# A triangular solve regrouped: four diagonal blocks of 8 rows and two levels of merging in place of two blocks of 16

## The chip, the cores and the metric

The kernel runs on one core of a Trainium2 chip. The metric is the device time of one launch in microseconds. The kernel before took 894.9 us, the median of three runs (891.95 to 898.2).

## What is computed

Three stages one after another: a delta-rule attention over 4 batches, 8 heads and 768 tokens of width 48, then a gated MLP without a nonlinearity, then a second MLP with SoLU and a layer norm.

```python
# attention, for each batch and head
k_n = k / (norm(k) + 1e-06)
for t in range(S):
    kt, vt, bt = k_n[t], v[t], beta[t]
    y[t] = q[t] @ state
    v_old = state.T @ kt
    state = state + bt * outer(kt, vt - v_old)
# first MLP:  x = ((x @ w1) * (x @ w2)) @ w3 @ w_out
# second MLP: h = x @ w_in; solu = h * softmax(h); layer norm * g; @ w_out
```

The loop over tokens is computed in chunks of 64 tokens. Inside a chunk the corrections of all tokens hang on one another through a lower triangular matrix, so each chunk needs the inverse of a unit lower triangular system. That inverse, made in halves of 32 rows, is what the change touches.

## The kernel before

**Tiles and groups.** The sequence is cut into six groups (NG = 6) of two chunks of 64 tokens. One group holds 32 systems (8 heads, 2 batch pairs, 2 chunks), and the two batches of a pair and the two 32-row halves of a chunk lie on the four quarters of the partitions. So one operation on a tile of 128 partitions by 32 x 32 elements works on the inverses of the whole group. Group 0 stands before the hardware loop, groups 1 to 4 are its two iterations of two groups, and group 5 stands behind it. In this attention stage the first MLP's products are already computed from the chunk before (`up` on TensorE, `keep_a` on ScalarE, `multiply` on VectorE), so they fill the engine between the steps of the recurrence.

**Two halves of a group.** Each group has two halves, one for each chunk (tt = 0 and tt = 1). On TensorE (`group`, L868) a half is: `k_state` (L767) for both pairs, `up` 0, `apply_inverse` of the first 32 rows, `up` 1, `cross_half`, `up` 2, `apply_inverse` of the second 32 rows, `up` 3, `outputs`, `up` 4, `add_state`, `up` 5, `outputs`, `up` 6, `add_state`, two `transpose_y`, `up` 7. In the first half the four `grams` of the next group stand between these. `k_state` waits at L772 for the semaphore `x_low` (written by `low_x`, L466, on VectorE), because it writes the PSUM banks from which `low_x` reads. `up` f waits at L847 for the `product` of `multiply` f-2. `apply_inverse` of the first half waits once a group for `inverse`.

**VectorE's queue.** It is written out by hand in `group` (L486): an engine works strictly in this order. In the first half it multiplies f = 0 to 3 and keeps the masked scores (`keep_pt`); behind the fourth `keep_pt` stand `coefficients` and `system_rows` of the next group's solve, and then the solve itself, cut into pieces between which the multiplications stand. In the first half these are rows 1 to 3, multiply 4, rows 4 to 6, multiply 5, rows 7 and 8, multiply 6, rows 9 and 10, both `low_x`, multiply 7; in the second half `right_hand`, rows 11 and 12, multiply 0, rows 13 to 15, multiply 1, `right_hand2`, and then the four pieces of merging and `stationary`, with multiplications 2 to 6 between, then both `low_x` and multiply 7. The solve of group 0 stands in one run before the groups (L573 to L579), and group 0 has no multiplications in its first half.

**The solve.** `system_rows` (L385) transposes the 32 x 32 Gram blocks (`amat`) and scales the rows with the coefficients `ci` and -1 (L390, 1024 elements). `substitute` (L394) solves two diagonal blocks of 16 rows at once: row i takes one product over 2 x i x i elements (L402) and one sum over them (L404), each waiting for the one before. `below_first` (L411) and `below_second` (L423) fill the lower left 16 x 16 block as -X22 A21 X11, in two parts each, of 1024 and 2048 products (L417, L429) with a sum behind each (L421, L433). In L429 the innermost index runs down a column of `xt`, in steps of 32 elements. `stationary` (L435) multiplies by `ci` (L439, 1024 elements) and transposes into `ti`, which `apply_inverse` reads.

Of the kernel before, what the change touches and what calls it, by code (L numbers as in the profile page):

```python
# [8 lines left out]
ALU = mybir.AluOpType  # L9
ACT = mybir.ActivationFunctionType  # L10
AX_X = mybir.AxisListType.X
# [5 lines left out]
P = 128  # L17
# [3 lines left out]
QB = HB // 2  # L21
NP = B // 2
# [72 lines left out]
def attention(nc, sb, sem, ps, m_dram, w34_dram, kq, ktok, vtok, beta, w1, w2, w3t, wo1,  # L95
# [11 lines left out]
    with ExitStack() as mem:  # L107
# [32 lines left out]

        zt = gd[:, 0:QB * QB // HB, :].rearrange("p s (a j) -> p (s a) j", j=QB)
        ksq = tmp[:, 0:SYS * D].rearrange("p (s d) -> p s d", d=D)
# [77 lines left out]

        GCOEF, GSOLVE = 4, 2 * (QB - 1) + 8 + 4

# [76 lines left out]
        def _(pool):  # L299
# [17 lines left out]
            const(pool.memset(xt[:, :, :].rearrange("p k j -> p (k j)")[:, 0:HB * HB:HB + 1], 1.0))  # L317
# [38 lines left out]
        def _(dve):  # L356
            def blocks(mat, first, *dims):

                a = mat[:, :, :]
                return bass.AP(a.tensor, a.offset + first, [list(a.ap[0]), [QB * HB + QB, 2], *dims])  # L360
# [48 lines left out]
            E8 = QB // 2  # L409

            def below_first(n, k0, j0, part):  # L411

                nj = QB - j0
                t = tmp[:, 0:QB * E8 * nj].rearrange("p (k i j) -> p k i j", k=E8, j=nj)
                step = GSOLVE * n + 3 + 2 * (QB - 1) + 2 * part
                dve.wait_ge(solve, step)
                dve.tensor_tensor(t, amat[:, QB:HB, j0:QB].unsqueeze(1).to_broadcast([P, E8, QB, nj]),  # L417
                                  xt[:, k0:k0 + E8, j0:QB].unsqueeze(2).to_broadcast([P, E8, QB, nj]),
                                  ALU.mult).then_inc(solve, 1)
                dve.wait_ge(solve, step + 1)  # L420
                dve.tensor_reduce(zt[:, k0:k0 + E8, :], t, AX_X, ALU.add).then_inc(solve, 1)  # L421

            def below_second(n, i0, nj, part):  # L423

                t = tmp[:, 0:QB * E8 * nj].rearrange("p (k i j) -> p k i j", k=QB, j=nj)
                x22 = xt[:, QB:QB + nj, QB + i0:QB + i0 + E8].rearrange("p j i -> p i j")
                step = GSOLVE * n + 3 + 2 * (QB - 1) + 2 * part
# [1006 lines left out]
```

## Time and profile before

| | us |
|---|---|
| median of three runs (lowest, highest) | 894.9 (891.95, 898.2) |
| span of the profiled execution | 894.6 |
| PE (TensorE matmul) busy | 819.3 |
| DVE (VectorE) busy | 524.4 |
| ACT (ScalarE) busy | 363.4 |
| POOL (GpSimd) busy | 62.9 |

Spans and starts are microseconds from the first instruction of the profiled execution. L402 is line 402 of the kernel. An idle time stands with the instruction that ends it, and with the one that released it. The attention stage reaches to about 540 us; groups 1 to 4 lie between 150 and 462 us.

### The profile page before, as it was taken

To read this page: it belongs to the slowest core of one execution; us is meant where nothing else is said; L and a number is where in the kernel's file an instruction comes from. 1 tells how busy PE (TensorE), PEld (TensorE's weight loads), DVE (VectorE), ACT (ScalarE), POOL (GpSimd) and SP (SyncE) were. 2 spreads that over 40 slices of the span, in tenths; PEclk is the share of its full clock that TensorE was granted. 3 is DMA by queue.
4 is the path that set the end of the run, shared out by engine and by line. 5 is a ranking of instruction groups with operands and counts; after the bars stand their busy time and mean duration, and the time that the engine had idled before them with its cause. 6 is when DMAs were issued, how large, how long until landed. Compare 5 with 4: busy or idle time off the path is not lost. (4 is left out here: it accounts for less than half of the span.)

```text
span 894.6 us, 22766 instructions
## 1 busy us (share of the span) xinstructions
PE 819.3 (92%) x9324; PEld 735.9 (82%) x9324; DVE 524.4 (59%) x859; ACT 363.4 (41%) x753; POOL 62.9 (7%) x102
## 2 busy tenths in 40 slices
PE   3869699999999899999999997999979999999995
PEld 2537588989889798988989996778869999999995
DVE  4794677379378837957872213444335566565663
ACT  2704522723453262354333323253334444444442
POOL 3410100010010001001000000000000000000000
PEclk9979888999899899999999999999999999999999
DMA  8772302220402221140011133756000000000000
GB/s 207 242 190 75 81 14 75 95 58 29 143 14 73 72 97 41 48 143 26 27 37 38 37 113 116 236 172 208 5 1 18 20 25 18 23 21 20 25 18 27
DMA packets 41226, 65.39 MB, mean 73 GB/s; under 512 B 3248, under 2 KB 31024, under 8 KB 39984
## 3 DMA queue, kind: packets, MB, share of 16 engines
q1 hardware_dynamic: 39120, 59.36, 22.6%
q10 hardware_dynamic: 2016, 4.72, 1.7%
q8 instruction: 70, 1.15, 0.5%
q14 instruction: 20, 0.16, 0.1%
HBM read 45.19 MB, written 18.87 MB: 72 GB/s over the span
## 5 line engine op out<-in xcount | busy, mean ns | idle before, releaser
L672 ACT COPY asb<-ps 128x256 f32<-128x256 f32 x96 | 35.7, 372 | 203.4 <-PE ps L852 203.1
L483 DVE TENSOR_TENSOR msb<-asb,ps 128x256 f32<-128x256 f32 x96 | 40.2, 419 | 91.0 <-ACT asb L672 90.6
L1361 PE MATMUL ps<-woh,uth 128*128 128x384 f32 x192 | 65.9, 343 | 2.6 <-DVE utl L1254 2.6
L852 PE MATMUL ps<-xh,w1h 128*128 128x256 f32 x288 | 61.4, 324 | 7.4 <-DVE msb L483 7.4
L1361 PE MATMUL ps<-woh,utl 128*128 128x384 f32 x192 | 65.8, 343 | 0.0
L1361 PE MATMUL ps<-wol,uth 128*128 128x384 f32 x192 | 65.6, 341 | 0.0
L1107 PE MATMUL ps<-mh,w34h 128*128 128x512 f32 x144 | 58.1, 403 | 7.0 <-DVE ml L1076 7.0
L763 PE MATMUL ps<-kqs,kbd 112*128 112x128 f32 x384 | 50.0, 287 | 12.3 <-ACT kbd L609 12.3
L763 PEld LDWEIGHTS ps<-kqs,kbd 112*128 112x128 f32 x384 | 48.4, 203 | 14.9 <-ACT kbd L609 13.8
L382 DVE TENSOR_TENSOR pt<-ps,mask 128x512 f32<-128x512 f32 x24 | 16.6, 690 | 71.9 <-ACT a L623 71.9
L1254 DVE TENSOR_TENSOR utl<-ps,uth 128x512 fp32r<-128x512 f32 x48 | 30.9, 686 | 45.2 <-ACT uth L1300 45.2
L1107 PE MATMUL ps<-ml,w34h 128*128 128x512 f32 x144 | 57.4, 399 | 0.0
L1107 PE MATMUL ps<-mh,w34l 128*128 128x512 f32 x144 | 57.3, 398 | 0.0
L1286 ACT ACTIVATE e<-ps,nmax 128x1024 f32<-128x1024 f32 x24 | 26.8, 1116 | 67.3 <-DVE nmax L1221 67.3
L852 PE MATMUL ps<-xh,w2h 128*128 128x256 f32 x288 | 52.6, 294 | 0.0
L852 PEld LDWEIGHTS ps<-xh,w1h 128*128 128x128 f32 x288 | 41.9, 196 | 12.5 <-DVE msb L483 7.9
L852 PE MATMUL ps<-xl,w2h 128*128 128x256 f32 x288 | 52.2, 292 | 0.0
L852 PE MATMUL ps<-xh,w1l 128*128 128x256 f32 x288 | 52.0, 291 | 0.0
L852 PE MATMUL ps<-xl,w1h 128*128 128x256 f32 x288 | 51.7, 290 | 0.0
L852 PE MATMUL ps<-xh,w2l 128*128 128x256 f32 x288 | 51.2, 288 | 0.0
L630 ACT COPY uu<-ps 32x384 f32<-32x384 f32 x96 | 45.1, 470 | 7.2 <-PE ps L789 5.8
L1227 DVE SCALAR_TENSOR_TENSOR u<-ps,e 128x1024 f32<-128x1024 f32 x24 | 29.4, 1224 | 31.8 <-ACT e L1286 31.8
(134 smaller groups left out, 1904.3 us busy)
## 6 DMA issues: line engine op xcount, KB each, us to landing
m_dram<-msb SPq DMA_DIRECT2D x48, 256.0 KB, 2.1
kqs<-in_kq SPq DMA_DIRECT2D x24, 384.0 KB, 6.2
mrest<-m_dram SPq DMA_DIRECT2D x36, 256.0 KB, 5.4
ks<-in_ktok SPq DMA_DIRECT2D x6, 768.0 KB, 7.7
vs<-in_vtok SPq DMA_DIRECT2D x6, 768.0 KB, 9.0
out<-osb SPq DMA_DIRECT2D x24, 192.0 KB
mfirst<-m_dram SPq DMA_DIRECT2D x12, 256.0 KB, 5.0
rr<-in_w SPq DMA_DIRECT2D x8, 192.0 KB, 4.4
```

Source lines behind the costliest of these rows:

```text
L382: dve.tensor_tensor(pt[:, par, tile, :, :], gbank[:, :, C:P], mask[:, :].unsqueeze(1).to_broadcast([P, H, C]), ALU.mult).then_inc(pt_made, 1)
L483: dve.tensor_tensor(msb[:, f // 2 % 2, f % 2, :], asb[:, f % 2, :], bbank[f % 2], ALU.mult).then_inc(product, 1)
L630: ins = act.copy(uu[rows, g, :], chain[g][rows, :])
L672: act.copy(asb[:, f % 2, :], abank[f % 2]).then_inc(a_kept, 1)
L763: ins = pe.matmul(gbank[:, h, :], kbd[:, tile % 2, h, :], kqs[:, par, tile, h, :], start=True, stop=True)
L852: ins = pe.matmul(bank, w[:, k, cols], xx[:, par, k, :], start=(j == 0 and k == 0), stop=(j == 2 and k == KD - 1))
L1107: ins = pe.matmul(hbank[par][k], w[:, f, k * P:(k + 1) * P], mm[:, u, f % UF, :, :].rearrange("p t c -> p (t c)"), start=(f == 0 and j == ...
L1227: dve.scalar_tensor_tensor(out=u[:, s, :], in0=hb[s], scalar=1.0, in1=e[:, :], op0=ALU.mult, op1=ALU.mult, accum_out=us[:, s:s + 1]).then_ ...
L1254: dve.tensor_tensor(utl[:, j, :, :], tb[j].rearrange("p (k c) -> p k c", c=P), uth[:, j, :, :].bitcast(F32), ALU.subtract).then_inc(ut_low, 1)
L1286: act.activation(e[:, :], hb[s], ACT.Exp, bias=nmax[:, s:s + 1], accum_out=es[:, s:s + 1]).then_inc(expd, 1)
L1361: ins = pe.matmul(ob, xx[:, j, k, :], w[:, 4 * j + k, :], start=(j == 0 and k == 0 and p == 0), stop=(j == 1 and k == 3 and p == 2))
```

## The change

The diagonal is solved in four blocks of 8 rows at once (`substitute` for rows 1 to 7, 4 x i x i elements each). Two new pieces, `eights_first` and `eights_second`, merge pairs of them to 16 rows; the merging to 32 rows stays. The sign moves into the sums (`negate=True`). The scaling by `ci` at the end (L439) is gone: `ci` is copied onto the diagonal of `xt` instead (32 elements), and the scaling at the start covers the diagonal 8 x 8 blocks only (256 elements). In `below_second` the products are laid out with the former inner index outside, so that the product reads in unit steps and the sum behind it reads in steps of 8 elements (32 bytes). GpSimd no longer writes ones onto the diagonal of `xt`. In VectorE's queue the pieces of the solve stand in other places: all seven rows, `eights_first` and `eights_second` now stand in the first half, ahead of both `low_x`, and rows 11 to 15 are gone from the second half.

```diff
 QB = HB // 2
+EB = QB // 2
...
         zt = gd[:, 0:QB * QB // HB, :].rearrange("p s (a j) -> p (s a) j", j=QB)
+        z8 = gd[:, 0:QB * QB // HB, :].rearrange("p s j -> p (s j)")[:, 0:QB * EB].rearrange(
+            "p (b k i) -> p b k i", b=2, k=EB)
...
-        GCOEF, GSOLVE = 4, 2 * (QB - 1) + 8 + 4
+        DIAG8, DIAG16 = EB * HB + EB, QB * HB + QB
+        MERGED8 = 4 + 2 * (EB - 1) + 7
+        GCOEF, GSOLVE = 4, MERGED8 + 8
...
             const(pool.memset(xt[:, :, :], 0.0))
-            const(pool.memset(xt[:, :, :].rearrange("p k j -> p (k j)")[:, 0:HB * HB:HB + 1], 1.0))
             const(pool.memset(st[:, :, :], 0.0))
...
             def system_rows(n):
+
                 dve.wait_ge(gram_kept, TPG * (n + 1))
                 dve.transpose(amat[:, :, :], gd[:, :, :].rearrange("p s i -> p i s")).then_inc(solve, 1)
+                if not static_below(n, 1):
+                    dve.wait_ge(inverse, n)
+                dve.wait_ge(solve, GSOLVE * n + 1)
+                dve.tensor_copy(steps_of(xt, 0, [HB + 1, HB]), ci[:, :]).then_inc(solve, 1)
                 dve.wait_ge(solve, GSOLVE * n + 2)
-
-                dve.scalar_tensor_tensor(out=amat[:, :, :], in0=amat[:, :, :], scalar=-1.0,
-                                         in1=ci[:, :].unsqueeze(2).to_broadcast([P, HB, HB]),
-                                         op0=ALU.mult, op1=ALU.mult).then_inc(solve, 1)
+                rows = steps_of(amat, 0, [DIAG8, HB // EB], [HB, EB], [1, EB])
+                dve.tensor_tensor(rows, rows, steps_of(ci, 0, [EB, HB // EB], [1, EB], [0, EB]),
+                                  ALU.mult).then_inc(solve, 1)
 
             def substitute(n, rows):
 
-
                 for i in rows:
-                    xs = blocks(xt, 0, [HB, i], [1, i])
-                    t = tmp[:, 0:2 * i * i].rearrange("p (b k j) -> p b k j", b=2, j=i)
-                    arow = blocks(amat, i * HB, [0, i], [1, i])
-                    dve.wait_ge(solve, GSOLVE * n + 3 + 2 * (i - 1))
+                    t = tmp[:, 0:4 * i * i].rearrange("p (b k j) -> p b k j", b=HB // EB, j=i)
+                    xs = steps_of(xt, 0, [DIAG8, HB // EB], [HB, i], [1, i])
+                    arow = steps_of(amat, i * HB, [DIAG8, HB // EB], [0, i], [1, i])
+                    dve.wait_ge(solve, GSOLVE * n + 4 + 2 * (i - 1))
                     dve.tensor_tensor(t, xs, arow, ALU.mult).then_inc(solve, 1)
-                    dve.wait_ge(solve, GSOLVE * n + 4 + 2 * (i - 1))
-                    dve.tensor_reduce(blocks(xt, i, [HB, i]), t, AX_X, ALU.add).then_inc(solve, 1)
-
...
+                    dve.wait_ge(solve, GSOLVE * n + 5 + 2 * (i - 1))
+                    dve.tensor_reduce(steps_of(xt, i, [DIAG8, HB // EB], [HB, i]), t, AX_X,
+                                      ALU.add, negate=True).then_inc(solve, 1)
+
+            def eights_first(n):
+
+                step = GSOLVE * n + 4 + 2 * (EB - 1)
+                t = tmp[:, 0:2 * EB * EB * EB].rearrange("p (b k i j) -> p b k i j", b=2, k=EB, j=EB)
+                dve.wait_ge(solve, step)
+                for b in range(2):
+                    at = b * DIAG16
+                    dve.tensor_tensor(t[:, b], steps_of(amat, at + EB * HB, [0, EB], [HB, EB], [1, EB]),
+                                      steps_of(xt, at, [HB, EB], [0, EB], [1, EB]), ALU.mult).then_inc(solve, 1)
+                dve.wait_ge(solve, step + 2)
+                dve.tensor_reduce(z8[:, :, :, :], t, AX_X, ALU.add).then_inc(solve, 1)
+
+            def eights_second(n):
+
+                step = GSOLVE * n + 4 + 2 * (EB - 1) + 3
+                t = tmp[:, 0:2 * EB * EB * EB].rearrange("p (b k j i) -> p b k j i", b=2, k=EB, j=EB)
+                dve.wait_ge(solve, step)
+                for b in range(2):
+                    x22 = steps_of(xt, b * DIAG16 + EB * HB + EB, [0, EB], [HB, EB], [1, EB])
+                    dve.tensor_tensor(t[:, b], x22, z8[:, b].unsqueeze(3).to_broadcast([P, EB, EB, EB]),
+                                      ALU.mult).then_inc(solve, 1)
+                dve.wait_ge(solve, step + 2)
+                for b in range(2):
+                    dve.tensor_reduce(steps_of(xt, b * DIAG16 + EB, [HB, EB], [1, EB]),
+                                      t[:, b].rearrange("p k j i -> p k i j"), AX_X, ALU.add,
+                                      negate=True).then_inc(solve, 1)
...
             def below_second(n, i0, nj, part):
 
-                t = tmp[:, 0:QB * E8 * nj].rearrange("p (k i j) -> p k i j", k=QB, j=nj)
-                x22 = xt[:, QB:QB + nj, QB + i0:QB + i0 + E8].rearrange("p j i -> p i j")
-                step = GSOLVE * n + 3 + 2 * (QB - 1) + 2 * part
+                t = tmp[:, 0:QB * EB * nj].rearrange("p (k j i) -> p k j i", k=QB, i=EB)
+                x22 = xt[:, QB:QB + nj, QB + i0:QB + i0 + EB]
+                step = GSOLVE * n + MERGED8 + 2 * part
                 dve.wait_ge(solve, step)
-                dve.tensor_tensor(t, x22.unsqueeze(1).to_broadcast([P, QB, E8, nj]),
-                                  zt[:, :, 0:nj].unsqueeze(2).to_broadcast([P, QB, E8, nj]),
+                dve.tensor_tensor(t, x22.unsqueeze(1).to_broadcast([P, QB, nj, EB]),
+                                  zt[:, :, 0:nj].unsqueeze(3).to_broadcast([P, QB, nj, EB]),
                                   ALU.mult).then_inc(solve, 1)
                 dve.wait_ge(solve, step + 1)
-                dve.tensor_reduce(xt[:, 0:QB, QB + i0:QB + i0 + E8], t, AX_X, ALU.add).then_inc(solve, 1)
+                dve.tensor_reduce(xt[:, 0:QB, QB + i0:QB + i0 + EB], t.rearrange("p k j i -> p k i j"), AX_X,
+                                  ALU.add, negate=True).then_inc(solve, 1)
 
             def stationary(n, par):
 
-                t = tmp[:, 0:HB * HB].rearrange("p (j i) -> p j i", i=HB)
-                dve.wait_ge(solve, GSOLVE * (n + 1) - 1)
-                dve.tensor_tensor(t, xt[:, :, :], ci[:, :].unsqueeze(2).to_broadcast([P, HB, HB]),
-                                  ALU.mult).then_inc(solve, 1)
                 dve.wait_ge(solve, GSOLVE * (n + 1))
                 dve.transpose(ti[:, par, :, :].rearrange("p s i -> p i s"),
-                              t.rearrange("p j i -> p i j")).then_inc(inverse, 1)
+                              xt[:, :, :].rearrange("p j i -> p i j")).then_inc(inverse, 1)
...
@@ -510,19 +537,18 @@
                     keep_pt(n + 1, nxt, 3)
                     coefficients(n + 1, nxt)
                     system_rows(n + 1)
-                    substitute(n + 1, range(1, 4))
                 if up0:
                     multiply(half, 4)
                 if ahead:
-                    substitute(n + 1, range(4, 7))
+                    substitute(n + 1, range(1, EB))
                 if up0:
                     multiply(half, 5)
                 if ahead:
-                    substitute(n + 1, range(7, 9))
+                    eights_first(n + 1)
                 if up0:
                     multiply(half, 6)
                 if ahead:
-                    substitute(n + 1, range(9, 11))
+                    eights_second(n + 1)
                 low_x(n, 0, 0)
...
                 right_hand(n, par, 1, 0)
                 right_hand(n, par, 1, 1)
-                if ahead:
-                    substitute(n + 1, range(11, 13))
                 multiply(half, 0)
-                if ahead:
-                    substitute(n + 1, range(13, QB))
                 multiply(half, 1)
                 right_hand2(n, 1, 0)
                 right_hand2(n, 1, 1)
                 if ahead:
-                    below_first(n + 1, E8, E8, 0)
+                    below_first(n + 1, EB, EB, 0)
                 multiply(half, 2)
                 if ahead:
                     below_first(n + 1, 0, 0, 1)
                 multiply(half, 3)
                 if ahead:
-                    below_second(n + 1, 0, E8, 2)
+                    below_second(n + 1, 0, EB, 2)
                 multiply(half, 4)
                 if ahead:
-                    below_second(n + 1, E8, QB, 3)
+                    below_second(n + 1, EB, QB, 3)
                 multiply(half, 5)
                 if ahead:
                     stationary(n + 1, nxt)
...
             system_rows(0)
-            substitute(0, range(1, QB))
-            below_first(0, E8, E8, 0)
+            substitute(0, range(1, EB))
+            eights_first(0)
+            eights_second(0)
+            below_first(0, EB, EB, 0)
             below_first(0, 0, 0, 1)
-            below_second(0, 0, E8, 2)
-            below_second(0, E8, QB, 3)
+            below_second(0, 0, EB, 2)
+            below_second(0, EB, QB, 3)
             stationary(0, 0)
```

## Rows read from the trace of the kernel before

**Rows 1.** Page, part 1: engine, busy us, share of the span, instructions
```profile
PE 819.3 (92%) x9324; PEld 735.9 (82%) x9324; DVE 524.4 (59%) x859; ACT 363.4 (41%) x753; POOL 62.9 (7%) x102
```

**Rows 2.** Waits of PE, 100 to 480 us: waiting <- releaser, total us, times, longest
```profile
PE ps L777 <- issue: 12.8, 3, 9.5
PE ps L852 <- DVE msb L483: 7.4, 4, 1.9
PE ps L777 <- DVE xl L470: 7.1, 4, 2.0
```

**Rows 3.** Timeline of PE: start, us, instruction, idle time before it and releaser
```profile
113.58 3.69 PE L777 MATMUL ps<-st,kqs 48*64 48x48 f32 x64 [9.50 <-issue]
...
149.88 2.65 PE L777 MATMUL ps<-st,kqs 48*64 48x48 f32 x64 [1.63 <-DVE xl L470]
...
187.42 0.62 PE L852 MATMUL ps<-xh,w1h 128*128 128x256 f32 x3 [1.86 <-DVE msb L483]
...
228.44 2.69 PE L777 MATMUL ps<-st,kqs 48*64 48x48 f32 x64 [1.75 <-DVE xl L470]
...
386.87 2.07 PE L777 MATMUL ps<-st,kqs 48*64 48x48 f32 x64 [1.75 <-DVE xl L470]
...
462.17 2.07 PE L777 MATMUL ps<-st,kqs 48*64 48x48 f32 x64 [1.72 <-issue]
```

**Rows 4.** Busy time by stretch: stretch, length, PE busy, granted clock, DMA share, GB/s
```profile
113.60:120.40 6.80, 6.80 (x79) 0.50 0.01 2
151.10:157.90 6.80, 6.80 (x54) 0.50 0.94 205
188.70:192.10 3.40, 3.40 (x43) 0.50 0.21 77
...
387.00:419.00 32.00, 32.00 (x578) 1.00 0.35 101
```

**Rows 5.** Timeline of DVE, first half of group 0
```profile
104.36 1.88 DVE L387 STREAM_TRANSPOSE amat<-gd 128x1024 f32<-128x1024 f32 x1
106.28 1.23 DVE L390 SCALAR_TENSOR_TENSOR amat<-amat,ci 128x1024 f32<-128x1024 f32 x1
...
112.93 1.01 DVE L470 TENSOR_TENSOR xl<-ps,xh 128x384 fp32r<-128x384 f32 x2
```

**Rows 6.** Groups of DVE instructions, shapes apart: xcount, busy us, mean ns, idle before
```profile
L429 DVE TENSOR_TENSOR tmp<-xt,gd 128x1024 f32<-128x1024 f32 x6 | 11.8, 1962 | 0.0
...
L421 DVE TENSOR_REDUCE gd<-tmp 128x128 f32<-128x1024 f32 x6 | 7.3, 1220 | 0.2
...
L404 DVE TENSOR_REDUCE xt<-tmp 128x14 f32<-128x98 f32 x6 | 1.5, 256 | 0.2
```

**Rows 7.** Timeline of DVE, first half of group 1
```profile
184.49 1.23 DVE L390 SCALAR_TENSOR_TENSOR amat<-amat,ci 128x1024 f32<-128x1024 f32 x1
...
186.94 0.42 DVE L483 TENSOR_TENSOR msb<-asb,ps 128x256 f32<-128x256 f32 x1
187.28 0.18 DVE L402 TENSOR_TENSOR tmp<-xt,amat 128x32 f32<-128x32 f32 x1
...
193.63 1.02 DVE L470 TENSOR_TENSOR xl<-ps,xh 128x384 fp32r<-128x384 f32 x2 [0.73 <-ACT xh L649]
```

**Rows 8.** Timeline of PE, between the halves of group 1 and in the second
```profile
194.98 2.07 PE L777 MATMUL ps<-st,kqs 48*64 48x48 f32 x64
...
203.16 1.55 PE L801 MATMUL ps<-uu,a 32*32 32x48 f32 x64
```

**Rows 9.** Timeline of DVE, second half of group 1
```profile
204.27 2.27 DVE L458 TENSOR_TENSOR rr<-rr,ps 32x384 f32<-32x384 f32 x4
...
224.14 1.22 DVE L439 TENSOR_TENSOR tmp<-xt,ci 128x1024 f32<-128x1024 f32 x1
```

**Rows 10.** Timeline of PE at the start of group 0
```profile
79.74 1.55 PE L789 MATMUL ps<-rr,ti 32*32 32x48 f32 x64
```

**Rows 11.** Timeline of DVE at the end of solve 0
```profile
71.84 2.09 DVE L442 STREAM_TRANSPOSE ti<-tmp 128x1024 f32<-128x1024 f32 x1
```

More of the change, by code:

```diff
@@ L356, in _, with steps_of @@
         def _(dve):
-            def blocks(mat, first, *dims):
-                a = mat[:, :, :]
-                return bass.AP(a.tensor, a.offset + first, [list(a.ap[0]), [QB * HB + QB, 2], *dims])
+            def steps_of(mat, first, *dims):
+                a = mat[:, :, :] if mat is not ci else mat[:, :]
+                return bass.AP(a.tensor, a.offset + first, [list(a.ap[0]), *[list(d) for d in dims]])
             def sum_squares(n):
@@ L402, in substitute @@
                     dve.tensor_tensor(t, xs, arow, ALU.mult).then_inc(solve, 1)
-                    dve.wait_ge(solve, GSOLVE * n + 4 + 2 * (i - 1))
-                    dve.tensor_reduce(blocks(xt, i, [HB, i]), t, AX_X, ALU.add).then_inc(solve, 1)
-            E8 = QB // 2
+                    dve.wait_ge(solve, GSOLVE * n + 5 + 2 * (i - 1))
+                    dve.tensor_reduce(steps_of(xt, i, [DIAG8, HB // EB], [HB, i]), t, AX_X,
+                                      ALU.add, negate=True).then_inc(solve, 1)
@@ L411, in below_first @@
             def below_first(n, k0, j0, part):
                 nj = QB - j0
-                t = tmp[:, 0:QB * E8 * nj].rearrange("p (k i j) -> p k i j", k=E8, j=nj)
-                step = GSOLVE * n + 3 + 2 * (QB - 1) + 2 * part
+                t = tmp[:, 0:QB * EB * nj].rearrange("p (k i j) -> p k i j", k=EB, j=nj)
+                step = GSOLVE * n + MERGED8 + 2 * part
                 dve.wait_ge(solve, step)
-                dve.tensor_tensor(t, amat[:, QB:HB, j0:QB].unsqueeze(1).to_broadcast([P, E8, QB, nj]),
-                                  xt[:, k0:k0 + E8, j0:QB].unsqueeze(2).to_broadcast([P, E8, QB, nj]),
+                dve.tensor_tensor(t, amat[:, QB:HB, j0:QB].unsqueeze(1).to_broadcast([P, EB, QB, nj]),
+                                  xt[:, k0:k0 + EB, j0:QB].unsqueeze(2).to_broadcast([P, EB, QB, nj]),
@@ L419, in below_first @@
                                   ALU.mult).then_inc(solve, 1)
                 dve.wait_ge(solve, step + 1)
-                dve.tensor_reduce(zt[:, k0:k0 + E8, :], t, AX_X, ALU.add).then_inc(solve, 1)
+                dve.tensor_reduce(zt[:, k0:k0 + EB, :], t, AX_X, ALU.add).then_inc(solve, 1)
             def below_second(n, i0, nj, part):
-                t = tmp[:, 0:QB * E8 * nj].rearrange("p (k i j) -> p k i j", k=QB, j=nj)
-                x22 = xt[:, QB:QB + nj, QB + i0:QB + i0 + E8].rearrange("p j i -> p i j")
@@ L427, in below_second @@
-                step = GSOLVE * n + 3 + 2 * (QB - 1) + 2 * part
+                t = tmp[:, 0:QB * EB * nj].rearrange("p (k j i) -> p k j i", k=QB, i=EB)
+                x22 = xt[:, QB:QB + nj, QB + i0:QB + i0 + EB]
+                step = GSOLVE * n + MERGED8 + 2 * part
                 dve.wait_ge(solve, step)
-                dve.tensor_tensor(t, x22.unsqueeze(1).to_broadcast([P, QB, E8, nj]),
-                                  zt[:, :, 0:nj].unsqueeze(2).to_broadcast([P, QB, E8, nj]),
+                dve.tensor_tensor(t, x22.unsqueeze(1).to_broadcast([P, QB, nj, EB]),
+                                  zt[:, :, 0:nj].unsqueeze(3).to_broadcast([P, QB, nj, EB]),
@@ L564, in _ @@
             dve.memset(kqs[32:64, 1, :, :, :], 0.0).then_inc(gap_zeroed, 1)
-            dve.wait_ge(consts, 9)
+            dve.wait_ge(consts, 8)
             dve.wait_ge(beta_in, 16)
@@ L727, in group @@
                         keep_a(half, 7)
-            act.wait_ge(consts, 9)
+            act.wait_ge(consts, 8)
             square(0, 1, 0)
@@ L911, in group @@
                     fill(tt, 7)
-            pe.wait_ge(consts, 9)
+            pe.wait_ge(consts, 8)
             for g in range(NP):
```

## The prediction

> **What bounds the kernel now.** I read the page first: PE is busy for 819.3 of 894.6 us and DVE for 524.4 [rows 1]. The change touches only DVE work, so it can move the end only where PE waits for DVE. The waits of PE in the attention stage are few: 12.8, 7.4 and 7.1 us in total, at `k_state` (L777) and at `up` (L852) [rows 2]. PE's timeline places them [rows 3]; I take each as a pause with the instruction behind it.
> - One pause of 9.50 us stands before `k_state` of the second half of group 0, at 113.58.
> - Between groups, before `k_state` of the next first half, there are five of 1.6 to 2.0 us (149.88, 228.44, 386.87 and 462.17 are shown). The releaser is `low_x`, the last thing behind the whole solve in DVE's queue. One more pause has no DVE behind it: of the 12.8 us of "issue" [rows 2], 9.50 and 1.72 are named here, and the 1.6 that are left stand where the hardware loop turns.
> - In the first half of groups 1 to 4 there are four of 1.86 us like that at 187.42, before `up` 6. It waits for multiply 4, which stands behind solve rows 1 to 3.
>
> Between the halves, where `low_x` stands at 193.63, DVE had sat idle for 0.73 us until ScalarE was ready [rows 7], and PE reached `k_state` at 194.98 with no pause [rows 8]. There the solve is hidden, with little to spare.
>
> PE's clock is the second thing to read. Behind a pause the granted clock is 0.50, that is 1.2 GHz instead of 2.4: for 6.8 us of work after the 9.50 us pause, 6.8 us after the one at 149.88, 3.4 us after the one at 187.42; from 387 to 419, after a pause of the same 1.75 us, it stayed at 1.00 [rows 4]. What this costs comes from two group periods. Group 1 takes 228.44 - 149.88 = 78.56 us with pauses of 1.75 + 1.86 and 6.8 + 3.4 = 10.2 us at the low clock; group 4 takes 462.17 - 386.87 = 75.30 us with 1.72 + 1.86 and only 3.4 us [rows 3, 4]. Equal work gives 74.95 - 10.2c = 71.72 - 3.4c, so c = 0.475 us lost per us at the low clock, and 70.1 us of bare PE work in a group. The mean period of groups 1 to 4, less the loop's 1.6, is (462.17 - 149.88 - 1.6) / 4 = 77.7 us.
>
> **The prices.** DVE's time grows in a straight line: a sum over 98 elements takes 256 ns, one over 1024 takes 1220 [rows 6], so 1.04 ns an element and 154 ns beside. Dependent instructions follow one another after about 35 ns (106.28 - 104.36 - 1.88 is 40) [rows 5]. With these:
> - `system_rows`: the transpose stays (1.92 from start to start [rows 5]). The scaling of 1024 elements, 1.23, becomes 256 elements, 0.42 + 0.04 = 0.46. The diagonal copy of 32 elements costs 154 + 33 ns and the gap, 0.22. Its wait for `inverse` names DVE's own work of a group ago and costs nothing.
> - Rows 1 to 7 with 4 x i x i = 4 to 196 elements: products 1.68, sums 1.67, 14 gaps of 0.035: 3.84.
> - `eights_first`: two products of 512 (0.69 each, which overlap by 0.08, as independent instructions do at 187.28 [rows 7]) and a sum of 1024 (1.22): 2.60.
> - `eights_second`: two products of 512 and two sums of 512, 2.67 if a sum in steps of 8 elements costs as one in unit steps. The trace has no strided sum. The nearest row is L429, a product that reads one operand in steps of 32 elements: 1962 ns for 1024 against 1220, or 1.77 ns an element instead of 1.04 [rows 6]. At that price the two sums take 0.37 more each: 3.40. Nothing suggests a price below the unit one or above L429's.
> - `below_second`: the product loses L429's surcharge and the sum gains the same at the dear price: nothing. At the cheap price 0.74 + 1.5 us are saved, in the second half.
> - `stationary` loses L439, 1.22 + 0.03 [rows 9].
> - `negate` changes no count of elements: nothing. GpSimd's missing memset is of 32 elements at the start, where the transfers of the inputs set the pace: nothing.
>
> I take the dear price for the strided sum, since L429 is the one row of DVE that shows steps wider than one. The Trainium skill (SBUF — State Buffer, the note on "cachelines" in the section Door 1: The DMA port swizzle) says that SBUF is read in lines of 16 bytes, and that each access to a new line pays. L429's 128-byte steps agree; that 32-byte steps pay too no row shows, and by the page they do, which speaks for the dear sum below rather than the cheap one.
>
> **Where it lies: solve 0.** DVE ends it at 71.84 + 2.09 = 73.93, and PE applies the inverse at 79.74, without a pause before it [rows 10, 11]. Ending some 5 us earlier gives nothing.
>
> **Where it lies: first halves.** The solve's pieces ahead of `low_x` grow, although the whole solve shrinks. Group 0 has no multiplications there, so it is one run: 104.36 to 112.93 = 8.57 us before [rows 5]; after, 1.92 + 0.22 + 0.46 + 3.84 + 2.60 + 3.40 = 12.44 (11.71 cheap). The pause of 9.50 us becomes 13.4 (12.6): +3.9 (+3.1).
>
> In group 1, and so in 2 to 4: the transpose ends into L390 at 184.49 [rows 7]. After the change multiply 4 starts at 184.49 + 0.22 + 0.46 = 185.17 instead of 186.94, so `up` 6 starts at about 185.65 and its pause is gone (185.56 is where PE stood ready). Then 0.34 for the multiply (187.28 - 186.94), rows 1 to 7 until 189.35, multiply 5, `eights_first` until 192.29, multiply 6, and `eights_second` until 192.63 + 3.40 = 196.03. `k_state` follows the start of `low_x` by 0.73 (113.58 - 112.93 = 0.65 in group 0 [rows 3, 5]; I take a little more): 196.76, cheap 196.0. PE's own work between 185.56 and 194.98 is 9.42 - 1.86 - 3.4 x 0.475 = 5.96 us, so it would be ready at about 191.6. The 1.86 us pause turns into pauses of 196.76 - 185.56 - 5.96 = 5.2 us together (4.5 cheap), nearly all before `k_state`. What queues behind `low_x` on DVE (multiply 7, both `right_hand`) is late with it, but PE wants those later still.
>
> **Where it lies: second halves.** Rows 11 to 15 leave DVE, but they lay where DVE would else wait for `cross_half`: it starts at 203.16, its first pair is there after about half of 1.55, at 203.95, and `right_hand2` starts at 204.27 [rows 8, 9]. So only 0.3 comes from them, and 1.25 from L439; together 1.55 of a pause of 1.75. About 0.2 stays (nothing at the cheap price).
>
> **The sum.** After the change a group takes 70.1 + 5.2 + 0.2 = 75.5 us and what the clock takes. The two pauses that now draw the clock down become one of 5 us; of the pauses in the trace a long one was followed by the full 6.8 us at 1.2 GHz [rows 4], so I take 6.8 x 0.475 = 3.2: 78.7 against 77.7, +1.0 a group, +4.0 for four. Group 0: +3.9 - (1.63 - 0.2) = +2.4, with its low clock as before. Group 5 has no solve. 894.6 + 6.4 = 901.0 us; the profiled execution and the median, 894.9, differ by 0.3, which I neglect.
>
> **The rivals.**
> - *Cheap strided sum, same clock.* A group takes 70.1 + 4.5 + 3.2 = 77.8 us, +0.1; group 0 +3.1 - 1.6 = +1.5; together about +2: 896.5 us. For it: a sum reads one stream, L429 two. Against it: nothing in the trace shows a free stride.
> - *The clock stays up, so it gets faster.* With the pause between groups gone, the loads that follow it (DMA share 0.94 from 151 to 158 [rows 4]) meet a PE that has not paused. If the 5 us pause too leaves the clock at 1.00, as the 1.75 us pause at 386.87 did, a group takes 75.5: 4 x -2.2 + 2.4 = -6.4, 888.2 us, and with cheap sums 884. It turns faster than before once the clock takes under about 1.6 us a group. Against it: of the four pauses whose clock is shown, three were followed by the low one [rows 4].
> - *The clock falls twice a group.* If the small rest of pauses still draws 3.4 us at another place, each group costs 1.6 more: 901.0 + 6.4 = 907.4 us. For it: pauses of only 1.86 us did this.
> - *Nothing moves.* If the late `low_x` is worth as much as the two pauses taken away, 894.9 us. That is the change not reaching PE at all; the sum is a difference of such terms, so it lies within their error.
>
> **How the numbers follow.** Chances: the forecast 0.40; cheap sums 0.25; clock stays up 0.12; falls twice 0.13; nothing moves 0.10. The range is 889 to 907: from the clock rival's dear case to the twice falling one, leaving out about half of each. About 1%, 9 us, is what a measurement can tell here. Slower by more (over 904): most of the double fall and a small part of the forecast, 0.19. Faster by more (under 886): the clock rival with cheap sums, 0.06. Within: 0.75.
>
> **What the profile after would show.** Right: a pause of about 13 us before `k_state` of group 0's second half; pauses of 4 to 5 us between the halves of groups 1 to 4, released by `low_x`; none at `up` 6 and nearly none between groups; sums of 1024 and 2048 elements in `below_second` at 1.96 and 3.8 us. Wrong would be sums at 1.22 and 2.28, a granted clock of 1.00 after the new pause, or substitution rows dearer than their element count says, as each adds straight to `low_x`.

## The result and the profile after

The changed kernel takes 906.15 us (median of four runs, 905.02 to 908.41) against 896.55 us for the kernel before in the same comparison: a ratio of 1.0117, 95% interval 1.0083 to 1.0151. It is slower by about 9.6 us. The forecast was 901.0 us in a range of 889 to 907: the time lies in the range and the sign is right, but the forecast put three chances in four on a change within 1%, and 1.2% it became. Of the 5.15 us above the forecast 1.65 are the kernel before, which it started from at 894.9; the change was forecast at +6.1 us and is +9.6.

VectorE's work did shrink. Its busy time fell from 524.4 us [rows 1] to 509.5, while the span of the profiled execution grew from 894.6 to 906.7:

```profile
span 906.7 us, 22668 instructions
...
PE 822.4 (91%) x9324; PEld 737.6 (81%) x9324; DVE 509.5 (56%) x805; ACT 363.7 (40%) x753; POOL 65.9 (7%) x101
```

PE's timeline shows where the pauses are now. Columns are start, duration, instruction, and in brackets the idle time before it and its releaser. L801 is `k_state`, which was L777:

```profile
118.89 3.73 PE L801 MATMUL ps<-st,kqs 48*64 48x48 f32 x64 [13.43 <-issue]
...
154.15 2.07 PE L801 MATMUL ps<-st,kqs 48*64 48x48 f32 x64 [0.55 <-DVE xl L497]
...
197.28 3.65 PE L801 MATMUL ps<-st,kqs 48*64 48x48 f32 x64 [4.17 <-issue]
...
312.31 1.71 PE L801 MATMUL ps<-st,kqs 48*64 48x48 f32 x39 [1.96 <-issue]
315.44 1.52 PE L801 MATMUL ps<-st,kqs 48*64 48x48 f32 x25 [1.41 <-issue]
...
359.21 3.65 PE L801 MATMUL ps<-st,kqs 48*64 48x48 f32 x64 [4.16 <-issue]
...
473.62 2.07 PE L801 MATMUL ps<-st,kqs 48*64 48x48 f32 x64 [0.51 <-issue]
```

Against [rows 3]: the 9.50 us pause of group 0 is 13.43, the 1.86 us pauses at `up` 6 are gone, the ones between groups are 0.5 but for the one at the turn of the hardware loop (312.31), which keeps its 2.0, and between the halves of groups 1 to 4, where PE never stopped before [rows 8], it stops for 4.16 us each time. `k_state` runs for 3.65 us behind the long pauses and 2.07 behind the short ones: that is the granted clock, 1.2 and 2.4 GHz.

The cause stands in VectorE's queue, first half of group 1, ahead of `low_x` (L497) at 196.63:

```profile
186.04 0.41 DVE L510 TENSOR_TENSOR msb<-asb,ps 128x256 f32<-128x256 f32 x1
...
190.24 0.41 DVE L510 TENSOR_TENSOR msb<-asb,ps 128x256 f32<-128x256 f32 x1
190.57 1.29 DVE L421 TENSOR_TENSOR tmp<-amat,xt 128x512 f32<-128x512 f32 x2
191.89 1.22 DVE L424 TENSOR_REDUCE gd<-tmp 128x128 f32<-128x1024 f32 x1
193.03 0.41 DVE L510 TENSOR_TENSOR msb<-asb,ps 128x256 f32<-128x256 f32 x1
193.35 1.29 DVE L433 TENSOR_TENSOR tmp<-xt,gd 128x512 f32<-128x512 f32 x2
194.68 2.04 DVE L437 TENSOR_REDUCE xt<-tmp 128x64 f32<-128x512 f32 x2
196.63 1.01 DVE L497 TENSOR_TENSOR xl<-ps,xh 128x384 fp32r<-128x384 f32 x2
```

Multiply 4 (186.04) is early enough for `up` 6 now. But VectorE works with no gap over 0.2 us up to `low_x`, where it had 0.73 us to spare before [rows 7]; `eights_first` and `eights_second` are 5.7 of the last 6.1 us. In the second half the same engine waits 3.66 and 3.23 us for ScalarE before multiplies 0 and 1, where rows 11 to 15 used to lie:

```profile
205.19 0.42 DVE L510 TENSOR_TENSOR msb<-asb,ps 128x256 f32<-128x256 f32 x1 [3.66 <-ACT asb L696]
208.85 0.42 DVE L510 TENSOR_TENSOR msb<-asb,ps 128x256 f32<-128x256 f32 x1 [3.23 <-ACT asb L696]
```

### The profile page after: what moved, and what is told of

Same layout as the page of the kernel before. It is cut to its first block and busy times, and to the rows that moved or that the text cites. A ratio compares the mean times of both kernels' runs of the same rounds, so it can differ in the third digit from the quotient of the medians.

```text
span 906.7 us, 22668 instructions
## 1 busy us (share of the span) xinstructions
PE 822.4 (91%) x9324; PEld 737.6 (81%) x9324; DVE 509.5 (56%) x805; ACT 363.7 (40%) x753; POOL 65.9 (7%) x101
## 3 DMA queue, kind: packets, MB, share of 16 engines
q1 hardware_dynamic: 39120, 59.36, 22.3%
## 5 line engine op out<-in xcount | busy, mean ns | idle before, releaser
L801 PE MATMUL ps<-st,kqs 48*64 48x48 f32 x768 | 33.1, 255 | 35.6 <-issue 34.0
L801 PEld LDWEIGHTS ps<-st,kqs 48*64 48x64 f32 x768 | 31.6, 171 | 38.2 <-issue 38.0
L787 PEld LDWEIGHTS ps<-kqs,kbd 112*128 112x128 f32 x384 | 48.5, 204 | 13.8 <-ACT kbd L633 12.7
```

The source lines that it names most:

```text
L787: ins = pe.matmul(gbank[:, h, :], kbd[:, tile % 2, h, :], kqs[:, par, tile, h, :], start=True, stop=True)
L801: ins = pe.matmul(chain[g][64 * bb:64 * bb + C, hc(h)], kqs[r, par, tile, h, 0:C], st[r, g, hc(h)], start=True, stop=True)
```

## The ledger that the experiments share

I compare one stretch in all profiles: from where PE stands ready before `k_state` of group 0's second half to the start of `k_state` in group 5. It holds every pause of PE that the changes move. For each kernel I add up PE's pauses over 0.2 us in it, and PE's busy time while the granted clock is 0.50, that is 1.2 GHz; what is left is stretch - pauses - 0.475 x work at the low clock, with the price c = 0.475 of the prediction, which came from two groups of the kernel before and was not fitted again.

| kernel | median us | PE ready at | stretch | pauses | work at 1.2 GHz | what is left |
|---|---|---|---|---|---|---|
| before | 896.6 | 104.1 | 358.1 | 27.3 | 38.7 | 312.4 |
| changed | 906.15 | 105.5 | 368.2 | 35.6 | 40.5 | 313.3 |
| e1_eights_late | 869.8 | 104.4 | 334.7 | 13.8 | 14.2 | 314.1 |
| e2_strided_products | 906.4 | 101.8 | 370.3 | 36.0 | 46.6 | 312.2 |
| e3_no_strides | 894.35 | 101.1 | 359.9 | 30.0 | 37.3 | 312.2 |
| e4_before_rows_early | 922.8 | 103.3 | 383.9 | 43.2 | 61.0 | 311.7 |
| e5_fold_only | 881.1 | 105.3 | 343.4 | 20.7 | 20.2 | 313.1 |
| e6_before_reordered | 882.4 | 105.5 | 342.1 | 20.2 | 18.3 | 313.2 |
| e7_order_by_slack | 864.8 | 101.9 | 328.5 | 9.2 | 13.0 | 313.0 |
| e8_second_late | 876.6 | 102.3 | 340.8 | 19.6 | 14.6 | 314.2 |
| e9_fold_reordered | 870.1 | 102.3 | 334.1 | 14.5 | 13.0 | 313.4 |
| e10_changed_again | 906.5 | 104.2 | 368.6 | 36.4 | 40.1 | 313.2 |

The stretch ranges over 55 us and what is left over 2.5. So in all these kernels the stretch is PE's own work plus pauses plus low clock. The changed kernel's extra 10.1 us in it are 8.3 us of pauses, 0.9 of clock and 0.9 that this count does not place. Outside the stretch, the point at which PE stands ready moves between 101.1 and 105.5 us from profile to profile (105.5 and 104.2 for the changed kernel itself), and what follows takes 430.5 to 435.1; differences of a few microseconds in the medians can come from there.

## Experiments

The queue theory: what costs is the work that stands ahead of `low_x` in the first half, through a pause of PE and the low clock behind it. The rival, the price theory: the strided sums and the added operations cost too much in themselves.

**The merging of the eights moved behind the waiting steps.**

```diff
-                if ahead:
-                    eights_first(n + 1)
                 if up0:
                     multiply(half, 6)
-                if ahead:
-                    eights_second(n + 1)
                 low_x(n, 0, 0)
                 low_x(n, 0, 1)
+                if ahead:
+                    eights_first(n + 1)
...
                 right_hand(n, par, 1, 0)
                 right_hand(n, par, 1, 1)
+                if ahead:
+                    eights_second(n + 1)
                 multiply(half, 0)
```

> The changed kernel with eights_first moved behind both low_x of the first half and eights_second behind both right_hand of the second. No operation is added or removed. Queue theory (the loss is what stands ahead of low_x in VectorE's queue): low_x in group 0 starts 6.0 us earlier, the 4.16 us pauses of groups 1 to 4 vanish or stay under 0.5, and the low clock that follows them goes at least in part; a group then takes 71 to 75 us instead of 79.9, and the whole 866 to 882 us, also below the kernel before (896.6). Price theory (the strided sums and the extra operations cost too much in themselves): VectorE's work is the same, so 902 to 908 us.

Measured: 869.8 us, ratio to before 0.9704 (0.966 to 0.9747). Not an operation less, and 36 us faster than the changed kernel, 25 faster than before. In PE's timeline the pauses between the halves of groups 1 to 4 are gone; group 0's is 7.02, those between groups 0.56, and at the turn of the loop two of 2.26 and 2.37 stay:

```profile
111.38 3.71 PE L801 MATMUL ps<-st,kqs 48*64 48x48 f32 x64 [7.02 <-issue]
...
219.02 2.07 PE L801 MATMUL ps<-st,kqs 48*64 48x48 f32 x64 [0.56 <-DVE xl L497]
```

The period from one `k_state` to the next group's, 147.60 to 219.02, is 71.4 us, where the changed kernel needs 78.4 (154.15 to 232.54). The price theory falls: every strided sum and every added operation is still there.

**The stride in the products instead of the sums.**

```diff
-                t = tmp[:, 0:QB * EB * nj].rearrange("p (k j i) -> p k j i", k=QB, i=EB)
-                x22 = xt[:, QB:QB + nj, QB + i0:QB + i0 + EB]
+                t = tmp[:, 0:QB * EB * nj].rearrange("p (k i j) -> p k i j", k=QB, j=nj)
+                x22 = xt[:, QB:QB + nj, QB + i0:QB + i0 + EB].rearrange("p j i -> p i j")
...
-                dve.tensor_reduce(xt[:, 0:QB, QB + i0:QB + i0 + EB], t.rearrange("p k j i -> p k i j"), AX_X,
-                                  ALU.add, negate=True).then_inc(solve, 1)
+                dve.tensor_reduce(xt[:, 0:QB, QB + i0:QB + i0 + EB], t, AX_X,
+                                  ALU.add, negate=True).then_inc(solve, 1)
```

and the same in `eights_second`.

> The changed kernel with the index order of before in eights_second and below_second: the products read a column of xt in steps of 32 elements, the sums read in unit steps. Queue theory with equal prices for both strides: products of 512 at 1.06 us instead of 0.69, sums the other way round, so low_x moves by at most 0.1 us and the time is within 2 us of the changed kernel (904 to 908). Price theory (a strided sum is dearer than a strided product): 3 us or more faster.

Measured: 906.4 us, the same as the changed kernel. The groups of DVE instructions (count, busy us, mean ns) of the changed kernel and then of this one show that the price only changes places:

```profile
L463 DVE TENSOR_REDUCE xt<-tmp 128x128 f32<-128x2048 f32 x6 | 23.8, 3960 | 0.2
...
L459 DVE TENSOR_TENSOR tmp<-xt,gd 128x2048 f32<-128x2048 f32 x6 | 13.8, 2305 | 0.0
...
L463 DVE TENSOR_REDUCE xt<-tmp 128x128 f32<-128x1024 f32 x6 | 12.5, 2080 | 0.2
L437 DVE TENSOR_REDUCE xt<-tmp 128x64 f32<-128x512 f32 x12 | 12.3, 1064 | 0.2
```

```profile
L459 DVE TENSOR_TENSOR tmp<-xt,gd 128x2048 f32<-128x2048 f32 x6 | 22.8, 3800 | 0.0
L463 DVE TENSOR_REDUCE xt<-tmp 128x128 f32<-128x2048 f32 x6 | 13.7, 2286 | 0.2
L433 DVE TENSOR_TENSOR tmp<-xt,gd 128x512 f32<-128x512 f32 x12 | 12.3, 1068 | 0.1
```

A strided sum of 2048 costs 3960 ns and a strided product 3800; the pause between the halves is 4.03 us instead of 4.16. That the medians agree to 0.3 us is in part chance: in its profile PE stands ready 3.6 us earlier, and the stretch is 2.1 us longer, mostly because behind the pauses of 4.03 us the low clock covers 8.1 to 8.7 us of work, against 6.6 to 8.5 in the changed kernel.

**The stride's price taken away.**

```diff
-                                      t[:, b].rearrange("p k j i -> p k i j"), AX_X, ALU.add,
+                                      t[:, b], AX_X, ALU.add,
```

and to the same effect in `below_second`.

> The changed kernel with the sums of eights_second and below_second reading the products in unit steps although these lie in the other index order, so the inverse that it computes is another matrix; everything else is as it was. This takes away the price of the stride alone. The two sums of 512 should take 1.3 us together instead of 2.04, so low_x in the first half comes 0.75 us earlier, in group 0 too, and the sums of below_second save 0.9 and 1.7 us, which closes the 0.55 us pause between groups. Queue theory: 5 x 0.75 + 5 x 0.55 = about 6 us faster, 899 to 901, still slower than before. If the strides are the whole loss: 896 or below.

Measured: 894.35 us (ten runs, 893.23 to 899.62), ratio 1.0011 (0.9986 to 1.0036). That is 11.8 us under the changed kernel where about 6 were expected, and no longer slower than before. The pause between the halves is 3.40 instead of 4.16 and the one between groups is gone, as worked out, but for 1.60 at the turn of the loop; in the ledger that is 5.6 us less of pauses, 1.5 of clock, and a stretch shorter by 8.3. The other 3.5 us lie outside it: in the profiles PE stood ready at 101.1 us here, in the changed kernel at 105.5 and 104.2. That point hangs on when the last pieces of `w3t` land: before it PE pauses for 5.4 to 8.9 us, released by a DMA, in every profile. Whether the stride has a part in it stays open, and the ten runs fall into six of 893.2 to 894.7 and four of 897.8 to 899.6, so the median itself can shift by some microseconds. The cheap rival's arithmetic (896.5 us) was right in kind. But this does not make the strides the cause of the loss. The kernel before reads strides too, in the products of L429, and of the strides taken away here only those of `eights_second` are new and stand ahead of `low_x` (0.75 us); and e1_eights_late keeps them all and takes 869.8 us.

**The order alone, made worse in the kernel before.**

```diff
-                    substitute(n + 1, range(9, 11))
+                    substitute(n + 1, range(9, 15))
                 low_x(n, 0, 0)
...
-                if ahead:
-                    substitute(n + 1, range(11, 13))
                 multiply(half, 0)
                 if ahead:
-                    substitute(n + 1, range(13, QB))
+                    substitute(n + 1, range(15, QB))
```

> The kernel before with rows 11 to 14 of the substitution moved from the second half to ahead of low_x in the first (4.2 us of VectorE work, the arithmetic untouched). Queue theory: group 0 loses 4.2 us, and in groups 1 to 4 k_state comes 2.8 us later, so 12 to 18 us slower than before (908 to 915), with a pause of some 3 us between the halves and the 1.86 us pause at up 6 kept. If the place of the solve in the queue does not matter: 895 to 898.

Measured: 922.8 us, ratio 1.0308 (1.0265 to 1.0351): 27.5 us slower with the arithmetic of before. The place alone is shown to be enough for a loss. The loss is more than the 12 to 18 expected, and the ledger says why: 15.9 us of pauses, as reckoned, and 22.3 us more of work at 1.2 GHz, worth 10.6, which I had left out. In PE's timeline there are now three pauses a group, these two and one of 1.6 us between groups:

```profile
188.80 0.62 PE L850 MATMUL ps<-xh,w1h 128*128 128x256 f32 x3 [1.87 <-DVE msb L483]
...
198.20 3.65 PE L775 MATMUL ps<-st,kqs 48*64 48x48 f32 x64 [3.16 <-issue]
```

**A middle dose.** Only `eights_second` goes behind `right_hand`; `eights_first` stays ahead of `low_x`.

```diff
-                if ahead:
-                    eights_second(n + 1)
                 low_x(n, 0, 0)
...
                 right_hand(n, par, 1, 1)
+                if ahead:
+                    eights_second(n + 1)
                 multiply(half, 0)
```

> The changed kernel with eights_second alone moved behind right_hand of the second half; eights_first stays ahead of low_x. A middle dose: the pause between the halves should fall from 4.16 to about 0.9 us. Queue theory without the clock: 5 x 3.3 = 16 us under the changed kernel, 889 to 891. With the clock (so short a pause no longer draws it down): another 10 to 14 us, 875 to 881.

Measured: 876.6 us, ratio 0.9789 (0.9741 to 0.9836), 29.5 us under the changed kernel. The pause is 0.89 us, as worked out, and by the ledger 16.0 us of pauses and 12.3 of clock are gone. Over 140 us of groups 1 and 2 (columns: stretch, length, PE busy, granted clock, DMA share, GB/s) the clock does not fall once, in the changed kernel it does; first this kernel, then the changed one:

```profile
150.00:290.00 140.00, 137.65 (x2470) 1.00 0.27 76
```

```profile
150.00:290.00 140.00, 130.57 (x2211) 0.95 0.27 75
```

**The fold alone.** Of the change only the scaling by way of the diagonal, with blocks of 16 rows in the places and the index order of before; the diff is against the changed kernel and shows the scaling alone.

```diff
-                rows = steps_of(amat, 0, [DIAG8, HB // EB], [HB, EB], [1, EB])
-                dve.tensor_tensor(rows, rows, steps_of(ci, 0, [EB, HB // EB], [1, EB], [0, EB]),
+                rows = steps_of(amat, 0, [DIAG16, 2], [HB, QB], [1, QB])
+                dve.tensor_tensor(rows, rows, steps_of(ci, 0, [QB, 2], [1, QB], [0, QB]),
                                   ALU.mult).then_inc(solve, 1)
```

> Of the change only the scaling folded into the diagonal (and the sign in the sums): the two blocks of 16 rows, the index order and the places in VectorE's queue are those of before. The scaling at the start covers 512 elements instead of 1024 and L439 of before (1.25 us) is gone. Queue theory: the pause at up 6 falls from 1.86 to about 1.3 us, the one between groups from 1.75 to about 0.5, so a group takes 72 us and 1.6 to 5 for the low clock: 876 to 888 us, faster than before by 8 to 20. Rival (savings of 2 us of VectorE work do not reach TensorE): 893 to 897.

Measured: 881.1 us, ratio 0.9819 (0.9767 to 0.987). VectorE is busy for 10.2 us less over the six solves (514.2 instead of 524.4), 1.7 a group, one part ahead of multiply 4 and the other at the end of the second half, and that gives 14 us. The pauses at `up` 6 are 1.3 to 1.7 us and those between groups 0.55, but for 1.87 at the turn of the loop. In the ledger 6.6 us of pauses and 8.8 of clock are gone.

**The order alone, made better in the kernel before.**

```diff
                     system_rows(n + 1)
-                    substitute(n + 1, range(1, 4))
                 if up0:
                     multiply(half, 4)
                 if ahead:
-                    substitute(n + 1, range(4, 7))
+                    substitute(n + 1, range(1, 7))
...
-                if ahead:
-                    substitute(n + 1, range(9, 11))
                 low_x(n, 0, 0)
                 low_x(n, 0, 1)
+                if ahead:
+                    substitute(n + 1, range(9, 11))
```

> The kernel before, with its arithmetic untouched: multiply 4 goes ahead of rows 1 to 3, and rows 9 and 10 go from ahead of low_x to behind it. Tells how much of what e1_eights_late gained (869.8 us) belongs to the order and how much to the changed arithmetic. Queue theory: the four pauses of 1.86 us at up 6 go, group 0 gains 1.5, the 1.75 us between groups stay, with the low clock behind them or not: 875 to 887. If the order gives all, 870; if the arithmetic gives all, 893 to 897.

Measured: 882.4 us, ratio 0.9841 (0.9794 to 0.9888). Order alone gives 12.7 us. The pause at `up` 6 is 0.54, not zero, and the 1.75 us between groups stay; behind them the low clock covers less work than before (18.3 us in the stretch instead of 38.7).

**Both, still with blocks of 16 rows.** The fold of e5_fold_only with the order of e6_before_reordered; the diff is against e5_fold_only.

```diff
                     system_rows(n + 1)
-                    substitute(n + 1, range(1, 4))
                 if up0:
                     multiply(half, 4)
                 if ahead:
-                    substitute(n + 1, range(4, 7))
+                    substitute(n + 1, range(1, 7))
...
                 low_x(n, 0, 0)
                 low_x(n, 0, 1)
+                if ahead:
+                    substitute(n + 1, range(9, 11))
```

> e5_fold_only with the order of e6_before_reordered: blocks of 16 rows, the scaling folded, multiply 4 ahead of the substitution, rows 9 and 10 behind low_x. Against e1_eights_late (869.8 us) it tells what the blocks of 8 are worth once the order is good. Queue theory (work that does not stand ahead of a waiting step is worth nothing): pauses of 0.5 us or none at up 6 and 0.5 between groups, 868 to 873, the same as e1_eights_late. Rival (the shorter solve counts wherever it stands): the 16-row substitution is some 2 us longer a group, so 878 or more.

Measured: 870.1 us, ratio 0.9717 (0.9648 to 0.9786); e1_eights_late, with blocks of 8, has 869.8 (0.9704). So with the merging of the eights behind `low_x` the blocks of 8 are worth nothing that can be measured: the gain of e1_eights_late over the kernel before is had with the fold and the order alone. That holds for these two orders. Blocks of 16 in the order of the next experiment, which also fills VectorE's waits in the second half, were not tried.

**The order that the slack suggests.** e1_eights_late, with the first part of `below_first` ahead of multiply 1, and rows 5 to 7 behind `low_x` in group 0; the diff is against e1_eights_late.

```diff
                 multiply(half, 0)
+                if ahead:
+                    below_first(n + 1, EB, EB, 0)
                 multiply(half, 1)
                 right_hand2(n, 1, 0)
                 right_hand2(n, 1, 1)
-                if ahead:
-                    below_first(n + 1, EB, EB, 0)
...
-                    substitute(n + 1, range(1, EB))
+                    substitute(n + 1, range(1, EB if up0 else 5))
...
                 if ahead:
+                    if not up0:
+                        substitute(n + 1, range(5, EB))
                     eights_first(n + 1)
```

> e1_eights_late, and in addition the first part of below_first goes ahead of multiply 1, into the 1.8 us that VectorE idles there (3.8 in group 0), and in group 0 rows 5 to 7 go behind low_x. Queue theory: the 0.55 us pauses between groups go (5 x 0.5), and k_state of group 0's second half starts 2 us earlier: 864 to 868 us, 2 to 5 faster than e1_eights_late. If TensorE is by now held by something else: 869 to 871.

Measured: 864.8 us, ratio 0.9647 (0.9602 to 0.9692). It beats both kernels: 3.5% faster than before, 4.6% than the changed one (864.8 / 906.15 = 0.954). Of PE's pauses over 0.2 us in the stretch these are left:

```profile
106.83 3.67 PE L803 MATMUL ps<-st,kqs 48*64 48x48 f32 x64 [4.96 <-issue]
...
284.42 1.33 PE L803 MATMUL ps<-st,kqs 48*64 48x48 f32 x39 [2.10 <-issue]
287.94 1.52 PE L803 MATMUL ps<-st,kqs 48*64 48x48 f32 x25 [2.18 <-issue]
```

The last two stand where the hardware loop turns, and the profile names no engine that they wait for.

**The changed kernel once more.**

> The changed kernel as it is, profiled again beside the kernel before. Tells which parts of its first profile repeat: the pauses of VectorE's making (4.16 between the halves, 0.55 between groups, 13.4 in group 0) should repeat within 0.05 us, and so should the time of 904 to 908; open is whether 10.2 us at the low clock in group 3 repeat (then they belong to the pause) or not (then to chance), and whether TensorE stands ready for group 0's second half at 105.5 us again or 1 to 4 us earlier.

Measured: 906.5 us, ratio 1.0118 (1.0044 to 1.0192). The pauses are 13.81 (0.4 more than in the first profile, where at most 0.05 was expected), 0.57 and 4.16 us, and the long low clock of group 3 is there again: behind the same pause 8.3 us of work at 0.50, in the first profile 8.5 (359.21 to 367.67). So it repeats with this kernel and does not look like chance. Why it is longer there than the 6.6 to 6.8 us behind the other pauses of 4.16 us stays open:

```profile
358.50:366.90 8.40, 8.38 (x100) 0.50 0.60 127
```

## Why the prediction was right or wrong

**Right: the mechanism.** That the pieces ahead of `low_x` grow while the solve shrinks, and that the loss lies between the halves. Ahead of `low_x` in group 0 the forecast was 12.44 us and the pause 13.4; it is 118.24 - 105.75 = 12.49 and 13.43. The profile names no releaser for the long pauses; that `low_x` ends them is read from the starts, `k_state` 0.65 us behind it in group 0 and in group 1, and from the experiments that move it. The pauses at `up` 6 are gone. Between groups 0.5 us stayed where 0.2 was forecast: the last sums are dearer than reckoned. At the turn of the loop nothing was gained: 1.96 us stayed of 2.00 (312.31, against 307.24 before).

**Right: the dear price of the strided sum.** 1064 ns for 512, 2080 for 1024, 3960 for 2048, a little above what L429 showed (1962 for 1024 [rows 6]). The Trainium skill (SBUF — State Buffer, the note on "cachelines" in the section Door 1: The DMA port swizzle) said that each access to a new 16-byte line pays; that a step of 32 bytes pays as much as one of 128 is now shown by e2_strided_products, where the two trade places and the price goes with them (3960 and 3800 ns).

**Slightly off: the pauses.** The forecast has 5.2 us of them in the first half of a group; 4.16 are there. The copy and the scaling start before the instruction ahead of them has ended and take 186.04 - 185.59 = 0.45 us instead of 0.68, `eights_first` took 193.03 - 190.57 = 2.46 us instead of 2.60 and `eights_second` 196.63 - 193.35 = 3.28 instead of 3.40, and `k_state` follows `low_x` by 0.65 instead of 0.73. That is 0.6 of the 1.0 us; the rest I can't place. The other way go the 0.3 us a group between groups and 1.8 us at the turn of the loop. Over the stretch 9.6 us of added pauses were forecast (2.4 in group 0 and 1.8 in each of four groups) and 8.3 measured.

**Wrong: the term of the clock.** "The two pauses that now draw the clock down become one of 5 us ... so I take 6.8 x 0.475 = 3.2." By the same numbers the kernel before pays 77.7 - 70.1 - 3.6 = 4.0 us a group, so this step credited the change with 0.8 us a group, 3.2 in all. By the granted clock of the profiles the low-clock work of groups 1 to 4 is 34.1 us in the changed kernel and 31.9 in the kernel before: no credit, but a cost of 1.0 us. The step took one fall of 6.8 us a group, 27.2 in all. It left out the fall at the turn of the loop, which is in the kernel before as well (5.3 us of work there, 5.4 after), and behind the pause at 359.21 the low clock covers 8.5 us of work; e10_changed_again repeats both (5.1 and 8.3). So over the stretch the sum was 9.6 of pauses less 3.2 of clock, 6.4 us; measured are 8.3 of pauses, 0.9 of clock and 0.9 not placed, 10.1 us. The pauses came out smaller than forecast, and without that the miss would have been larger. The rival "falls twice a group", priced at 907.4 us, was right for group 3 alone. Its reason was not: it blamed the small rests of pauses, but behind the pauses of 0.55 to 0.9 us in e8_second_late the clock stayed up. That its price lies so near the measured time is luck.

**Not shown: one number of the price.** The price c = 0.475 took 3.4 us at the low clock in group 4, which no row shows. In the profile 2.83 us of work lie at 0.50 there (421.36 to 424.19), and with these the same two equations give c = 3.23 / (10.24 - 2.83) = 0.44, the value that also fits the twelve rows of the ledger best. It changes no reading above: the clock's terms shrink by a twelfth.

**Wrong: the chances.** With the clock term at zero the same sum gives 904 us, and the chance of "slower by over 1%" would, by my estimate, have been near one half instead of 0.19. I had spread chance over a gain (the clock rival, 0.12) that would have needed the 5 us pauses to leave the clock alone.

**Right: solve 0.** It ends earlier (69.57 us instead of 73.93), PE's wait for `w3t` lies beside it in every profile, and PE nowhere stops for it.

## What to carry to other kernels

In a queue that is written out by hand, ask of each piece what waiting step stands behind it; a shorter computation that is moved ahead of such a step can cost more than a longer one behind it. Look for the places where the engine waits for others anyway and put the independent work there: the same operations went from 906 to 865 us by order alone. And count a pause of TensorE with what the clock takes behind it: the 16.0 us of pauses that e8_second_late takes out of the changed kernel brought 12.3 us of clock with them.

## What the runs showed of the hardware that was not expected

- Short pauses left TensorE's clock alone and longer ones did not. Over groups 1 and 2 of e8_second_late (pauses of 0.89 and 0.56 us) the granted clock is 1.00. The pauses of 3.4 us in e3_no_strides and of 4.16 us in the changed kernel each came with 5.9 to 8.5 us of work at 0.50.
- In between it goes both ways. In the kernel before the clock fell at three of the five pauses between groups (1.6 to 2.0 us) and at all four of 1.86 us at `up` 6. In e6_before_reordered, where those at `up` 6 are down to 0.54, it fell at three of five too, but for half as long where the loop does not turn (3.4 instead of 6.8 us). In e5_fold_only the two pauses of 1.67 us at `up` 6 drew it down (the first three matmuls behind the pause take 1.01 us instead of 0.63) and the two of 1.33 us did not:

```profile
184.33 1.01 PE L879 MATMUL ps<-xh,w1h 128*128 128x256 f32 x3 [1.67 <-DVE msb L510]
...
257.98 0.63 PE L879 MATMUL ps<-xh,w1h 128*128 128x256 f32 x3 [1.33 <-DVE msb L510]
```

What decides in that middle range stays open.

- A sum that reads in steps of 32 bytes costs 1.73 times a sum in unit steps (3960 against 2286 ns for 2048 elements, the latter in e2_strided_products), and a product with one operand in steps of 128 bytes 1.65 times one in unit steps (3800 against 2305).
- The turn of the hardware loop comes with two pauses of PE, 2.10 and 2.18 us in e7_order_by_slack, with no releaser in the profile, and with 6.4 us of work at 0.50 behind them. In the kernel before the first of the two (2.00 us) has `low_x` as its releaser; in the changed kernel they are 1.96 and 1.41 us.
